# The last key chunk of each transposed probability tile at 64 columns, and a last token tile that two batches share

## What is computed

```python
def _attn_ref(q, k, v):                      # (4, 8, 576, 64) each
    scores = scale * np.matmul(q, k.transpose(0, 1, 3, 2))
    kth = np.partition(scores, -top_k, axis=-1)[..., -top_k:-top_k + 1]
    scores = np.where(scores >= kth, scores, -1000000000.0)
    attn = softmax(scores)
    return np.matmul(attn, v)

def _moe_ref(x, w_val, conv_w, w_out):       # conv over tokens, 5 taps
    gate = 1.0 / (1.0 + np.exp(-gate_pre))
    return (gate * (x @ w_val)) @ w_out

def _moe2_ref(x, w_ch1, w_ch2):
    X = np.fft.fft(np.fft.fft(x, axis=1), axis=2)
    u = x + np.real(X)
    un = (u - mu) / np.sqrt(var + 1e-06)
    return u + np.maximum(un @ w_ch1, 0.0) @ w_ch2
```

## Time and profile before

| | |
|---|---|
| time, median of 3 runs | 1050.89 us (1049.84 to 1052.85) |
| time of the profiled execution | 1052.33 us, of which the span is 1050.6 |
| PE busy | 972.2 us (93%) |
| DVE busy | 839.0 us (80%) |
| ACT busy | 647.2 us (62%) |
| POOL busy | 408.2 us (39%) |
| mean granted clock of PE | 0.963 of full speed |

### The profile page before, as it was taken

The page is one execution under the profiler, slowest core; times in us unless marked ns, Lnnn a source line. Parts: engine busy times, 40 slices in busy tenths (PEclk is TensorE's granted clock), DMA queues, the critical chain, the costliest instruction groups (busy, mean ns, idle before and its releaser), DMA issues.

```text
span 1050.6 us, 20124 instructions
## 1 busy us (share of the span) xinstructions
PE 972.2 (93%) x6784; PEld 831.6 (79%) x6784; DVE 839.0 (80%) x1824; ACT 647.2 (62%) x1421; POOL 408.2 (39%) x544
## 2 busy tenths in 40 slices
PE   4876767899999999999999999999999999999997
PEld 3555655678888898878898889878888888888896
DVE  7999999988999999989999977898999973120000
ACT  5887687856777767665777666666676762122121
POOL 2675544534533333244333332243442222543221
PEclk9997688799999999999999999999999999999999
DMA  9565656560186778511777655510676776059873
GB/s 237 181 202 167 220 185 200 173 215 24 26 293 228 284 265 293 177 35 34 274 269 259 200 202 198 163 35 24 214 262 244 261 252 231 1 199 358 297 248 129
DMA packets 84549, 203.80 MB, mean 194 GB/s; under 512 B 9056, under 2 KB 30304, under 8 KB 84448
## 3 DMA queue, kind: packets, MB, share of 16 engines
q1 hardware_dynamic: 84288, 202.22, 57.2%
q10 hardware_dynamic: 160, 0.30, 0.1%
HBM read 178.89 MB, written 23.59 MB: 193 GB/s over the span
## 4 chain that ended last, share of the span: by engine, by line
PE 77%; DVE 8%; issue 6%; ACT 6%; POOL 1%; DMA 0%; SPq 0%; ACTq 0%; DVEq 0%; POOLq 0%
PE p_m L757 18%; PE p_m L774 18%; PE p_t L604 9%; PE p_t L588 7%; PE p_s L574 7%; PE p_m L725 5%; PE p_m L647 4%; DVE rest L1004 3%; DVE top L993 3%; PE p_m L615 3%; PE p_m L706 3%; PE p_m L635 2%; PE p_t L608 2%; ACT prob L852 1%; ACT pT L866 1%
## 5 line engine op out<-in xcount | busy, mean ns | idle before, releaser
L993 DVE MAX8 top<-rest 128x8 f32<-128x576 f32 x432 | 310.3, 746 | 0.1
L1266 POOL TENSOR_TENSOR hid_lo<-hid,hid_hi 128x256 fp32r<-128x256 f32 (+1 forms) x128 | 107.5, 840 | 298.2 <-ACT hid_hi L934 298.2
L1004 DVE MATCH_REPLACE8 rest<-top,rest 128x576 f32<-128x576 f32 x288 | 214.1, 744 | 0.0
L774 PE MATMUL p_m<-w_st,hid_hi 128*128 128x512 f32 x576 | 181.3, 396 | 1.6 <-ACT hid_hi L934 0.7
L757 PE MATMUL p_m<-un_hi,w_st 128*128 128x256 f32 (+1 forms) x1024 | 164.2, 303 | 0.0
L840 ACT ACTIVATE s_sb<-p_s 128x576 f32<-128x576 f32 x144 | 93.1, 647 | 105.5 <-PE p_s L574 105.3
L757 PEld LDWEIGHTS p_m<-un_hi,w_st 128*128 128x128 f32 x1024 | 143.5, 188 | 5.6 <-issue 1.9
L588 PE MATMUL p_t<-id_sb,prob 128*128 128x128 f32 x720 | 111.6, 288 | 27.6 <-ACT prob L858 27.2
L933 ACT ACTIVATE hid<-p_m 128x256 f32<-128x256 f32 (+1 forms) x128 | 51.8, 405 | 128.5 <-PE p_m L757 127.6
L604 PE MATMUL p_t<-pT,v_sb 128*64 128x128 f32 (+1 forms) x1600 | 108.6, 288 | 22.9 <-ACT pT L866 22.9
L604 PEld LDWEIGHTS p_t<-pT,v_sb 128*64 128x64 f32 x1600 | 89.0, 149 | 48.6 <-ACT pT L866 29.6
(11 more groups left out here) (117 smaller groups left out, 1650.3 us busy)
## 6 DMA issues: line engine op xcount, KB each, us to landing
w_st<-w_split SPq DMA_DIRECT2D x256, 512.0 KB, 4.6
w_split<-w_st SPq DMA_DIRECT2D x32, 512.0 KB, 3.3
k_raw<-kT SPq DMA_DIRECT2D x62, 144.0 KB, 3.0
q_raw<-qT SPq DMA_DIRECT2D x60, 144.0 KB, 2.9
u<-w_ch SPq DMA_DIRECT2D x32, 256.0 KB, 3.9
v_sb<-v SPq DMA_DIRECT2D x16, 256.0 KB, 3.1
w_st<-wout_split SPq DMA_DIRECT2D x16, 256.0 KB, 3.9
out<-u SPq DMA_DIRECT2D x16, 256.0 KB, 2.4
```

Source lines behind the costliest of these rows:

```text
L774: mm = pe.matmul(mbank(j), h[i % 2][:, P * j:P * j + P], w2_st[i % NB2][:, w, :], start=f == 0 and part == 0, stop=f == FC - 1 and part == 2)
L993: found = dve.max(top[t % NK][:, 8 * n:8 * n + 8], (rest[t % 2] if n else s_sb[t % NS])[:, :])
L1004: chained(dve.match_replace(rest[t % 2][:, :], top[t % NK][:, 8 * n:8 * n + 8], (rest[t % 2] if n else s_sb[t % NS])[:, :], LOWEST), t)
L1266: pool.tensor_tensor(hid_lo[i % 2][:, 0:width(b, g)], hid[:, 0:width(b, g)], hid_hi[i % 2][:, 0:width(b, g)].bitcast(F32), ALU.subtract).t ...
```

## The change

Five things are changed.

1. In `transpose_p` the fifth transpose of every tile but the first takes 64 columns of `prob` and writes rows 0 to 63 of its 128 columns of `p_t`. Rows 64 to 127 keep the zeros that the first tile has left there. ACT still copies all 640 columns.
2. The last token tiles of batches 0 and 1, and those of 2 and 3, are projected, normalised and transposed together, with the odd batch. `STEPS` loses `proj 4` and `trn 4` for the even batch. POOL writes the even batch's transform into `u[4]` instead of `pm`, and in the odd batch DVE adds the projection to it with one more TENSOR_TENSOR of 64x512. The steps of the even batches spread anew over their slots, and the wait for the last transpose moves from `ch0` 12 to `ch0` 10.
3. Around the end of batch 0's attention: the first two `val` steps begin in slots 35 and 37 instead of 39, half a convolution moves from slot 41 to 39, the last half comes after the first `val` in slot 42, and ACT takes the last tanh of batch 0 after the exponentials of that slot and not before them.
4. The convolution on DVE of the last pair is cut in three ranges (384, 128 and 64 tokens) instead of two (384 and 192).
5. At the start two of the four loads of head 1 are issued by ACT instead of SP, and the low part of the first queries is made on DVE instead of POOL.

```diff
 def steps_by_slot():
-        steps = [(what, b, n) for what, n in STEPS]
+        steps = [(what, b, n) for what, n in STEPS if b % 2 or (what, n) not in LAST_TILE]
...
-CONV0_AT = {14: (0, 0), 16: (0, 1), 23: (1, 0), 25: (1, 1), 32: (2, 0), 34: (2, 1), 41: (3, 0), 42: (3, 1)}
-CONV_LAST = max(CONV0_AT)
+CONV0_AT = {14: (0, 0), 16: (0, 1), 23: (1, 0), 25: (1, 1), 32: (2, 0), 34: (2, 1), 39: (3, 0), 42: (3, 1)}
...
-VAL0_AT, VAL0 = 39, 2
+VAL0_AT = {35: 0, 37: 1}
...
                 def transpose_p(t):
...
-                        mm = pe.transpose(p_t[:, c * P:c * P + P], prob[t % 3][:, c * P:c * P + P], id_sb[:, :])
+
+                        m = REST if c == NCH - 1 and t else P
+                        mm = pe.transpose(p_t[0:m, c * P:c * P + P], prob[t % 3][:, c * P:c * P + m], id_sb[:, :])
...
                 def make_u(b, r):
...
+                    at, made = slice(0, P), us(b) + 2 * (r + 1)
+                    if r == NR - 1:
+
+                        at, made = rows(b, r), us(b + 1)
+                        early = rows(b - 1, r)
+                        dve.tensor_tensor(u[r][early, :], y[early, :], u[r][early, :], ALU.add).then_inc(m_u, 1)
...
                 dve.wait_ge(s_hi, 1)
                 dve.tensor_tensor(k_lo[0][0][:, :], k_raw[:, :], k_hi[0][0][:, :].bitcast(F32),
                                   ALU.subtract).then_inc(s_lo[0], 1)
+                dve.wait_ge(s_hi, 2)
+                dve.tensor_tensor(q_st[0][0][0:D, 0:S], q_raw[0:D, :], q_st[0][0][0:D, 0:S].bitcast(F32),
+                                  ALU.subtract).then_inc(s_lo[0], 1)
```

More of the change, by code:

```diff
@@ L85, in un_cols @@
     return slice(c0, c0 + ROWS[r][1])
+TRANSPOSED = [10, 12]
 def hidden_bank(b, g, f):
     if g == 0:
-        return 3 if f == 1 or f >= 12 and f % 2 == 0 else 2
+        return 3 if f == 1 or f >= TRANSPOSED[b % 2] and f % 2 == 0 else 2
     return 2 if (b % 2 == 0 or f == 1) and f % 2 else 3
@@ L116 @@
 NORM_AT = {("proj", 1): 0, ("proj", 2): 1, ("ch0", 1): 2, ("ch0", 4): 3, ("ch0", 7): 4}
+LAST_TILE = [("proj", NR - 1), ("trn", NR - 1)]
 COST = {"val": 2.2, "zed": 3.0, "seq": 2.6, "proj": 2.9, "trn": 0.6, "ch0": 3.1}
@@ L394, in folded, with tile_cols @@
             return gate[:, c, o * HALF + P * m:o * HALF + P * m + P]
[L396 to L401, removed]
+        def tile_cols(r):
+            return slice(ROWS[r][0], ROWS[r][0] + P)
         def w_out_half(b, k, h):
@@ L518, in _ @@
                     sp.dma_start(k_raw[D * half:D * half + D, :], kT[0, 0]).then_inc(s_qk_in[0], 16)
-                load_qk(0, 1)
+                for half in range(2):
+                    sp.dma_start(raw(0, 1)[0][D * half:D * half + D, :], qT[0, 1]).then_inc(s_qk_in[1], 16)
                 sp.wait_ge(s_zero, FILLS)
@@ L650, in value_products, with early_values @@
                     return mm
-                def early_values():
+                def early_values(j):
                     pe.wait_ge(m_wval, 16)
                     pe.wait_ge(s_feat_ev, KC)
-                    for j in range(VAL0):
-                        value_products(0, j, range(KC - 1))
+                    value_products(0, j, range(KC - 1))
                 def values(b, j):
@@ L672, in values @@
                         pe.wait_ge(m_tanh, KC)
-                    value_products(b, j, range(KC - 1 if b == 0 and j < VAL0 else 0, KC)).then_inc(m_val, 1)
+                    value_products(b, j, range(KC - 1 if b == 0 and j in VAL0_AT.values() else 0, KC)).then_inc(m_val, 1)
                 def zed(b, m):
@@ L724, in project @@
                             for c0, c1, w in w_out_half(b, k, h):
-                                mm = pe.matmul(bank[:, c0:c1], x[:, k, gv_cols(b, r)], w, start=n + k == 0,
+                                mm = pe.matmul(bank[:, c0:c1], x[:, k, tile_cols(r)], w, start=n + k == 0,
                                                stop=n == 2 and k == KC - 1, skip_group_check=True)
@@ L808, in _ @@
                         attend(s - ATTEND)
-                    if s in CONV0_AT and s != CONV_LAST:
+                    if s in CONV0_AT:
                         convolve(*CONV0_AT[s])
-                    if s == VAL0_AT:
-                        early_values()
+                    if s in VAL0_AT:
+                        early_values(VAL0_AT[s])
                     for x in plan[s][1:]:
@@ L937, in _ @@
                     act.dma_start(q_raw[D * half:D * half + D, :], qT[0, 0]).then_inc(s_qk_in[0], 16)
+                for half in range(2):
+                    act.dma_start(raw(0, 1)[1][D * half:D * half + D, :], kT[0, 1]).then_inc(s_qk_in[1], 16)
                 high_keys(0, 0)
@@ L946, in _ @@
                         store_pT(s - TRANSPOSE)
-                    if s in TANH0_AT:
+                    if TANH0_AT.get(s, KC - 1) < KC - 1:
                         gate_tanh(0, TANH0_AT[s])
@@ L965, in _ @@
                         store_out(s - ATTEND)
+                    if TANH0_AT.get(s) == KC - 1:
+                        gate_tanh(0, KC - 1)
                     for b, c in tanh_due(s):
@@ L1057, in conv @@
                     n0, n1 = part
-                    dve.wait_ge(s_x, 5 * p + (3 if part == FRONT else 5))
+                    dve.wait_ge(s_x, 5 * p + {FRONT: 3, NEXT: 4}.get(part, 5))
                     if c == 0:
@@ L1072, in make_u @@
                     g = [0, 0, 1, 1, 2][r]
-                    at = rows(b, r)
                     lo, hi = (1, 0) if r in (1, 3) else (0, 1)
@@ L1117, in step @@
                         finish(b, int(what == "ch1"))
-                    if (what, n) in NORM_AT:
+                    if (what, n) in NORM_AT and outs(b) + NORM_AT[what, n] < outs(b + 1):
                         normalise(b, NORM_AT[what, n])
```

104 lines of the change are left out of this document (53 added, 51 removed).

## The result

The changed kernel takes 1053.42 us (median of 20 runs, 1050.48 to 1058.56), the kernel before 1049.86 (20 runs beside it, 1046.02 to 1052.85). The ratio is 1.0042, 95% interval 1.0030 to 1.0055: slower by 4.4 us, 3.2 to 5.8. That is outside the predicted range of 1055 to 1077, on its lower side. The sign was right, and nearly everything that had led to it was not.

What follows compares the result with a forecast made beforehand. DVE was taken to bound batch 0's searches, PE and DVE alternate stretches after, PE the end; 19.6 + 3.0 + 0.8 - 3.0 - 0.3 - 2.6 - 0.7 = +16.8 us, set slightly lower at 1067 us, range 1055 to 1077.

Steps and rivals of the forecast that it cites:

- Part 1, +23.4 us before the waits and the clock: Array shape changes around each tile's fifth transpose: +19.6 us in PE's stretches, +3.0 and +0.8 in DVE's.
- so I take 0.35 us: Price per tile of the fifth transpose's change to 128*64 and back, read around `attend`; ends 0 and 0.38 us.
- Rival A: The 64 column transpose pays no price for changing the array's shape; 1044 us, chance 0.12.
- PE can give 4.8 us of waiting and the 3.5 us that part 2 frees: DVE stretch 268 to 455 us: PE's room absorbs most of 11.2 us added work, about +3.0 comes through.
- rival C: Nothing is absorbed: PE's waits stay and all 105 round trips count, 36.8 us; 1077 us, chance 0.13.
- Part 2, "changes no sum": Even batches' steps moving a slot here and there cost nothing; only -0.3 us, from the odd batch's `trn 4`.
- Rival D: Even batches' projections one slot later make DVE wait, at most 6 us on top; 1073 us, chance 0.10.
- The clock, -3.0: Near 453 and 692 us, filled PE waits for `gv` avoid the lower clock that follows them: -3.0 us.
- Part 3, -2.6: End of batch 0: DVE's 2.56 us wait for the first `val` goes, -2.6 us; ends 0 and -4.
- nothing that PE saves or loses there counts: From 10 to 205 us batch 0's searches on DVE alone set the pace, so PE's work has no effect.
- Part 5, -0.7: Start: low part of the first queries on DVE lets the first search begin earlier, -0.7 us, 0 to -1.3.

Runs made afterwards that it cites:

- e9: The kernel before with each tile's fifth transpose written as a plain f32 matmul with 64 columns of weights: 1092.4 us, ratio 1.0408.
- e10: The kernel before with the fifth transpose written as a plain f32 matmul at full width, 128 columns: 1059.63 us, ratio 1.0092.
- e5: The changed kernel with ACT doing the exponentials ahead of the first hidden chunk's evictions: ratio 0.9999 to the kernel before.
- e8: The changed kernel with ACT's exponentials first, POOL's low part of head 1's queries a slot later, and PE's later wait for `un_lo`: ratio 1.0000 to the kernel before.
- e2: The kernel before with the shared last token tile (part 2) alone: 1057.28 us, ratio 1.0083.
- e15: The kernel before with part 3 alone, run again: 1044.52 us, ratio 0.9951.
- e1: The kernel before with the 64 column fifth transpose (part 1) alone: ratio 1.0003, +0.3 us.
- e12: The kernel before with part 5 alone: ratio 1.0008, +0.8 us.
- e13: The kernel before with part 4 alone: ratio 1.0012, +1.3 us.
- e16: The kernel before with parts 1, 3, 4 and 5, all but part 2, run again: 1047.13 us, ratio 0.9982.
- e11: The kernel before with part 3 alone: 1043.83 us, ratio 0.9950, -5.2 us.

## Why the prediction was wrong

The parts measured alone add up: +0.3 (part 1), +8.7 (part 2), -5.2 (part 3), +1.3 (part 4), +0.8 (part 5) are +5.9 us, where the whole measures +4.4 (3.2 to 5.8). The prediction's sum of +16.8 had another make-up altogether.

- **Part 1, +23.4 us before the waits and the clock: measured +0.3.** This is the step that failed, and the words are "The transpose is nearest to `attend` and to the L682 of the earlier trace rows, so I take 0.35 us". The price had been read well: e9 pays 0.34 us. It was carried from an operation that pays it to one that doesn't. There was a row that spoke against it, the projection of the earlier trace rows, and it was set aside for its operands' type. The division that fits every row is by how the operation is issued, one instruction or a pair. None of the rows read showed a transpose at 128*64, and the prediction had 0 as one end of the price; it took too small a chance for it. Rival A had the mechanism right and 0.12.
- **"PE can give 4.8 us of waiting and the 3.5 us that part 2 frees", so only +3.0 of 11.2 would come through: wrong, but it had no price to act on.** e9 and e10 show that work added on PE between slots 53 and 71 counts in full, as rival C said (its 105 round trips of 36.8 us are 32.8 in e9 against e10), while e5 and e8 show that work taken away there doesn't count. My reading, which no run tests by itself, is that both engines are chains there: DVE waits for probabilities that PE and ACT make just in time, and PE's idle time stands where it has nothing to do yet.
- **Part 2, "changes no sum": measured +8.7 alone.** The prediction priced what the edit removed and went on; it never asked which wait the removed projection had covered. The earlier trace rows had the answer in sight: the projection is followed by L757, which reads `un_lo`. That PE would wait was not the costly half. In e5 POOL's 2.2 us are still there, and what is left of the cost is 0.4 and 1.4 us. ACT's evictions, queued ahead of the exponentials and dragged along by PE's wait, passed it on to DVE. Rival D spoke of the steps of even batches falling badly, at up to 6 us, but with another mechanism, a projection one slot later.
- **The clock, -3.0: not found.** The waits for `gv` near 453 and 692 did not go away (2.9 and 3.0 us in after), as there was no added work to fill them, and the granted clock is 0.57 from 448 to 452 us in after as it was from 454 to 458 before. From 692 to 728 the clock did come to 1.00 in the profile of after, but the new waits in batch 2 took it to half speed at 736 to 744 us. e2 has 0.89 over 32 us at both places.
- **Part 3, -2.6: measured -5.2, and -5.1 in e15.** The size was short by half, and -4 was the end that I gave. The mechanism holds only in part. DVE has no wait at all from 195 to 230 us in after, where before it had 2.56 us for `val`. But most of that wait is also gone in e1 and e12, which don't have part 3: there DVE waits 0.7 and 0.4 us for `val`. Up to the searches of tile 42, DVE in e12 and in e15 is equally far ahead of before, 4.9 us. Only behind them does part 3 show: at tile 50 it is 7.9 us in e15 and still 4.9 in e12. e12's waits of DVE, from 205 to 230 us and then from 230 to 268, that e15 doesn't have are

```profile
DVE gv L1116 <- PE p_m L648: 0.4, 1, 0.4
```

```profile
DVE rinv L1054 <- ACT prob L859: 1.5, 1, 1.5
DVE gv L1116 <- PE p_m L648: 0.5, 1, 0.5
```

  together 2.4 of these 2.9 us. The last section comes to the rest of part 3's 5 us, and to why "nothing that PE saves or loses there counts" fails.
- **Part 5, -0.7: measured +0.8 (-1.3 to +2.9).** The first copy of scores comes 0.3 us earlier in after, but no earlier in e12, part 5 alone. It is too small to be seen.
- **Rival A's time, 1044, was missed as well**, since with its price of zero there was nothing left to hide part 2. The sign of the forecast was right for a cause that it had priced at nothing.

## What to carry to other kernels

A price read between two operations belongs to those operations: before it is carried to a third, divide the rows that pay from the rows that don't by every property in which they differ, and if one property is left open, give "no price" the chance that it deserves. When a step is removed, look up what the step behind it waits for, and then what is queued behind that wait on the engines that follow; here 2.2 us on PE cost little until ACT's program order made them DVE's. Measure the parts of a bundle alone: this one held a gain of 5.2 us that the bundle turned into a loss of 4.4.

## What the runs showed of the hardware

- A transpose of f32 data with 64 columns of weights, between 128 column work, costs the same as one with 128 (0.109 us step, 0.46 us for the five, ratio 1.0003). The same operands as a plain f32 matmul cost 0.11 us a tile more at full width and 0.34 more again at 64 columns, which made 9.6 and 32.8 us of the whole, most of it behind slot 43. Behind a 64 column transpose a plain f32 step in 128*64 still starts 0.64 us after the transposes, as behind a full one.
- Batch 0's stretch, in which DVE is full and PE has a quarter of its time to spare, isn't free of PE all the same. From 150 to 205 us and from 205 to 230 the profiles show, for before, e12 and e15 in turn:

```profile
150.00:205.00 55.00, 41.05 (x278) 33.76 (x278) 54.12 (x113) 42.48 (x88) 30.10 (x37) 0.78 0.52 172
205.00:230.00 25.00, 23.13 (x156) 19.00 (x156) 21.03 (x51) 15.89 (x35) 8.66 (x12) 1.00 0.76 263
```

```profile
150.00:205.00 55.00, 40.51 (x309) 33.30 (x309) 55.00 (x116) 44.84 (x95) 30.83 (x39) 0.84 0.58 195
205.00:230.00 25.00, 23.93 (x154) 19.43 (x153) 24.23 (x58) 14.29 (x29) 8.05 (x11) 1.00 0.64 227
```

```profile
150.00:205.00 55.00, 41.59 (x326) 33.84 (x327) 55.00 (x116) 46.25 (x100) 31.86 (x40) 0.91 0.59 196
205.00:230.00 25.00, 24.20 (x161) 19.16 (x162) 24.90 (x63) 16.38 (x34) 8.20 (x12) 1.00 0.64 226
```

At a granted clock of 0.78 PE gets 278 instructions done from 150 to 205 us, at 0.84 309, and at 0.91, with part 3, 326. PE then comes to the end of batch 0 late or early, and DVE's busy time from 205 to 230 us is 21.0, 24.2 and 24.9 us. That is the 5 us by which e1 and e12 are ahead of before at slot 43 in the table: the execution that was profiled of before, 1052.33 us, is one of its longer ones, and the runs of before that stood beside e13 to e16 lie mostly near 1046.5 or near 1051.5, with few between. The clock of each run agrees: beside e13 to e16 the 17 runs up to 1047.6 us have a mean granted clock of 0.968 or more, the 17 above 1049.9 one of 0.966 or less.

What part 3 has to do with it is seen over all profiles. Of the eleven kernels with part 3, nine show a granted clock of 0.91 from 150 to 205 us, e8 0.87 and e5 0.84. Of the seven without it four show 0.78, e2 0.81, and e1 and e12 0.84. From 0.84 to 0.91 nothing more is gained up to tile 42, as e12 and e15 show. At 0.78 before and e13 are both 5 us later there. So an estimate of part 3's gain is the 2.9 us of its own and, as half of the runs of before are in the later group, half of 5 us: some 5.4, where 5.1 and 5.2 were measured. The estimate takes it that part 3 keeps its runs out of the later group. All six runs of e11 lie at 1042.7 to 1046.2 us, but two of the twelve of e15 at 1047.9 and 1049.0; and no run varied the clock alone. What lets it fall in some runs and not in others stays open. It also means that one pair of profiles can show 5 us that the change didn't make: by them alone, after had gained 9.7 us by slot 43.
